# Expert tiles that do not exist count nothing on any engine; the last MLP block holds the last 512 tokens in token order and is stored by plain transfers

## The reference

```
# 1. linear attention with a decaying state, per head h
state = gamma[h] * state + k_t^T v_t ;  y_t = (q_t @ state) / 8
# 2. mixture of experts, 8 experts, 512 -> 1024 -> 512, one expert per token
e = argmax(x @ w_gate)
out = softmax(x @ w_gate)[e] * sigmoid(x @ w_output_gate)[e] * (relu(x @ w1[e]) @ w2[e])
# 3. gated MLP on every token, 512 -> 1536 -> 512
xn = x / sqrt(mean(x*x) + 1e-6) * rms_g
result = (silu(xn @ w_gate) * (xn @ w_val)) @ w_out
```

## Time and profile before

| | us |
|---|---|
| timed runs, median (lowest to highest) | 1160.51 (1159.92 to 1163.32) |
| the profiled execution | 1156.39 |
| its span | 1154.6 |
| TensorE matmul busy | 1117.5, 97% of the span |
| VectorE, ScalarE, GpSimd busy | 437.6, 383.0, 166.0 |

### The profile page before, as it was taken

One profiled execution on the slowest core, in us unless ns is written; L12 is line 12 of the kernel. 1 busy time (PEld: TensorE's weight loads), 2 busy tenths in 40 slices (PEclk: granted clock), 3 DMA queues, 4 the chain that ended last, 5 costly groups with the idle time before them and its releaser, 6 DMA issues.

```text
span 1154.6 us, 19327 instructions
## 1 busy us (share of the span) xinstructions
PE 1117.5 (97%) x6051; PEld 936.4 (81%) x6052; DVE 437.6 (38%) x826; ACT 383.0 (33%) x631; POOL 166.0 (14%) x216
## 2 busy tenths in 40 slices
PE   7999999999999999998999999999999999999995
PEld 6999988787878887876888788888888888888884
DVE  4777755432414416331434323222332332333221
ACT  2455433443434436432241313213131321313111
POOL 2444423333311101110000100100010010001001
PEclk9999999999999999998999999999999999999998
DMA  9989814534334633422200200100010010000000
GB/s 206 254 231 241 215 56 155 178 114 127 109 109 139 207 109 110 159 81 90 84 26 1 74 1 1 73 0 0 0 73 0 0 73 0 0 0 37 1 1 36
DMA packets 111838, 97.24 MB, mean 84 GB/s; under 512 B 80640, under 2 KB 86192, under 8 KB 111792
## 3 DMA queue, kind: packets, MB, share of 16 engines
q1 hardware_dynamic: 97744, 66.07, 20.7%
q0 software_dynamic: 7648, 22.60, 5.5%
q10 hardware_dynamic: 6400, 7.96, 2.1%
HBM read 76.40 MB, written 20.21 MB: 84 GB/s over the span
## 4 chain that ended last, share of the span: by engine, by line
PE 52%; ACT 0%; DVE 0%; issue 0%; POOLq 0%; POOL 0%; ACTq 0%
PE bank L660 17%; PE bank L662 17%; PE bank L661 17%; PE bank L631 0%; DVE hl L1279 0%; ACT hh L936 0%; POOLq L97 0%; POOL out_rows L1446 0%; ACT more_rows L943 0%; POOLq L1450 0%; ACTq L935 0%; POOLq L1445 0%
## 5 line engine op out<-in xcount | busy, mean ns | idle before, releaser
L1270 DVE TENSOR_TENSOR gated<-bank,sig 128x512 f32<-128x512 f32 x72 | 49.8, 692 | 323.0 <-ACT sig L929 323.0
L660 PE MATMUL bank<-xh,w1h 128*128 128x512 f32 x384 | 149.4, 389 | 0.0
L661 PE MATMUL bank<-xl,w1h 128*128 128x512 f32 x384 | 149.4, 389 | 0.0
L662 PE MATMUL bank<-xh,w1l 128*128 128x512 f32 x384 | 149.4, 389 | 0.0
L929 ACT ACTIVATE sig<-bank 128x512 f32<-128x512 f32 x72 | 43.1, 598 | 289.7 <-PE bank L662 289.7
L660 PE MATMUL bank<-w2h,hh 128*128 128x512 f32 x288 | 113.2, 393 | 4.7 <-DVE hl L1279 4.7
L662 PE MATMUL bank<-w2h,hl 128*128 128x512 f32 x288 | 112.2, 390 | 0.0
L661 PE MATMUL bank<-w2l,hh 128*128 128x512 f32 x288 | 112.1, 389 | 0.0
L1088 DVE TENSOR_TENSOR hidl<-bank,hidh 128x512 fp32r<-128x512 f32 x58 | 39.8, 687 | 151.1 <-ACT hidh L804 151.1
L1446 POOL DMA_INDIRECT out_rows<-x_out,cur_idx x12 | 11.8, 982 | 591.1 <-ACT x_out L943 589.3
L936 ACT ACTIVATE hh<-prod 128x512 fp32r<-128x512 f32 x72 | 45.5, 632 | 154.2 <-PE bank L662 133.6
(11 more groups left out here) (214 smaller groups left out, 1966.8 us busy)
## 6 DMA issues: line engine op xcount, KB each, us to landing
stage<-in_moe_w SPq DMA_DIRECT2D x64, 512.0 KB, 5.3
expert_rows<-tile_o ACTq DMA_DIRECT2D x29, 256.0 KB
q_raw<-in_q SPq DMA_DIRECT2D x24, 256.0 KB, 5.5
k_raw<-in_k SPq DMA_DIRECT2D x24, 256.0 KB, 6.2
v_raw<-in_v SPq DMA_DIRECT2D x24, 256.0 KB, 3.5
yr<-expert_rows SPq DMA_DIRECT2D x5, 1024.0 KB, 5.7
stage<-in_moe_w_out SPq DMA_DIRECT2D x6, 512.0 KB, 3.3
stage<-in_moe_w_gate SPq DMA_DIRECT2D x5, 512.0 KB, 7.1
```

Of the source, the lines that this page charges most:

```text
L660: pe.matmul(out_ap, lh, rh, start=first, stop=False)
L661: pe.matmul(out_ap, lh, rl, start=False, stop=False)
L662: return pe.matmul(out_ap, ll, rh, start=False, stop=last)
L1270: v3.tensor_tensor(gated[:], bank[GV[f % 2][0]][:, :], sig[:], ALU.mult).then_inc(s["gated_done"], 1)
```

## The change

- **Tiles that do not exist.** TensorE and ScalarE lose their Else branches and count nothing for a missing tile. A third word of `flags`, `extra`, holds the number of real tiles beyond 24. Each waiter loads it and waits for `extra + SURE` tiles. ScalarE's result of the last real tile moves behind the loop. TensorE's first down product waits for `tile_out` (the bank has been read) in place of `tile_stored`.
- **Order of the rows in the MLP.** Blocks 0 to 4 hold the tokens of units 0 to 19, packed by expert; block 5 holds units 20 to 23 in token order. A row's place in `expert_rows` is now a third word of its metadata, and every block is fetched by four indirect DMAs of GpSimd (`fetch_y`, `fetch_late`) in place of plain ones. For block 0 these wait for 17 stored tiles in place of 13, and stand ahead of `fetch_rows(20)` in place of `fetch_rows(19)`.
- **Metadata.** 20 units are scattered in place of 24, two behind each of the fetches of tiles 6 to 15, and read back behind the fetch of tile 17 in place of tile 18. Routing gains four small VectorE instructions ahead of `control_ready`, three ahead of `gates_ready`, and two copies behind it.
- **Stores.** Blocks 0 to 4 are stored as before. Block 5 is stored by four plain DMAs of SyncE, one for each `sum_out`.

The diff, cut to its core:

```diff
-ROWS_FROM = SURE - 5
-FINAL_AFTER = 13
+ROWS_FROM = SURE - 4
+FINAL_AFTER = 17
...
-        meta_dram = nc.dram_tensor("row_meta", (TOKENS, 2), U32).ap()
+        meta_dram = nc.dram_tensor("row_meta", (LEAD_UNITS * P, 3), U32).ap()
...
-            def load_rows(n):
-                sp.wait_ge(s["xn_turned"], KD * n)
-                sp.dma_start(yr[:].bitcast(U32), y_dram[ds(n * BLK * P, BLK * P), :].rearrange("(t p) d -> p t d", p=P))\
-                  .then_inc(s["yrows_in"], 16)
-
-            sp.wait_ge(s["tile_stored"], 16 * TILES)
-            with sp.Fori(1, NBLK) as n:
-                load_rows(n)
+            extra = sp.value_load(flags[0:1, 2:3], min_val=0, max_val=TILES - SURE)
+            sp.wait_ge(s["tile_stored"], 16 * (extra + SURE))
+            sp.sem_inc(s["stood"], 1)
             for t in range(BLK):
-                sp.wait_ge(out_stored[t], 16 * NBLK)
+                sp.wait_ge(s["sum_out"], BLK * (NBLK - 1) + t + 1)
+                sp.dma_start(out[(LEAD_UNITS + t) * P:(LEAD_UNITS + t + 1) * P, :], out_rows(t))\
+                  .then_inc(s["late_stored"], 16)
+            sp.wait_ge(s["late_stored"], 16 * BLK)
+            for t in range(BLK):
+                sp.wait_ge(out_stored[t], 16 * (NBLK - 1))
...
-                with pe.Else():
-                    pe.wait_ge(s["tiles_done"], a + 1)
-                    pe.sem_inc(s["tiles_done"], 1)
...
+            extra = pe.value_load(flags[0:1, 2:3], min_val=0, max_val=TILES - SURE)
...
-                    pe.wait_ge(s["tile_stored"], 16 * TILES)
+                    pe.wait_ge(s["tile_out"], extra + SURE)
+                    pe.sem_inc(s["stood"], 1)
...
-                    act.wait_ge(s["rows0_in"], 32)
+                    act.wait_ge(s["rows0_in"], 16 * BLK)
                 else:
-                    act.wait_ge(s["yrows_in"], 16 * n)
...
-            def result_if_real(a):
-                with act.If(act.value_load(real[0:1, ds(a, 1)], min_val=0, max_val=1)):
-                    tile_result(a)
-                    store_tile(a)
-                with act.Else():
-                    act.wait_ge(s["tile_stored"], 16 * a)
-                    act.sem_inc(s["tile_stored"], 16)
...
                     expert_tile(a)
-                with act.Else():
-                    result_if_real(a - 1)
 
             with act.Fori(SURE, TILES - 1) as a:
                 tile_if_real(a)
             tile_if_real(TILES - 1)
-            result_if_real(TILES - 1)
+            extra = act.value_load(flags[0:1, 2:3], min_val=0, max_val=TILES - SURE)
+            tile_result(extra + SURE - 1)
+            store_tile(extra + SURE - 1)
...
-            settle(v3.tensor_tensor_scan(upto_n[:], scan_ones[:], n_e[:], 0.0, ALU.mult, ALU.add))
-            settle(v3.tensor_tensor(ahead_e[:], upto_n[:], n_e[:], ALU.subtract))
+            also(v3.tensor_tensor(early_n[:], lead_counts, ecap, ALU.subtract))
+            settle(v3.tensor_tensor_scan(upto_n[:], scan_ones[:], n_e[:], 0.0, ALU.mult, ALU.add), 2)
+            also(v3.tensor_tensor_scan(early_upto[:], scan_ones[:], early_n[:], 0.0, ALU.mult, ALU.add))
+            settle(v3.tensor_tensor(ahead_e[:], upto_n[:], n_e[:], ALU.subtract), 2)
+            also(v3.tensor_tensor(early_e[:], early_upto[:], lead_counts, ALU.subtract))
...
-            settle(v3.tensor_scalar(flags[:, 0:1], runs_f, -2.0, None, ALU.add), 6)
+            also(v3.tensor_scalar(flags[:, 2:3], end_e[0:1, EXPERTS - 1:EXPERTS], float(LEAD - SURE), None, ALU.add))
+            settle(v3.tensor_scalar(flags[:, 0:1], runs_f, -2.0, None, ALU.add), 7)
...
+                also(v3.tensor_tensor(order[:], onehot[:, 0:LEAD_UNITS, :],
+                                      early_e[:, :].unsqueeze(1).to_broadcast([P, LEAD_UNITS, EXPERTS]), ALU.mult))
                 settle(v3.tensor_tensor(back[:], onehot[:], back_e[:, :].unsqueeze(1).to_broadcast([P, UNITS, EXPERTS]),
-                                        ALU.mult), 2)
-                settle(v3.tensor_reduce(back_f[:], back[:], X, ALU.add))
-                settle(v3.tensor_tensor(meta_idx[:], slot_f[:], back_f[:], ALU.add))
+                                        ALU.mult), 3)
+                also(v3.tensor_reduce(order_f[:], order[:], X, ALU.add))
+                settle(v3.tensor_reduce(back_f[:], back[:], X, ALU.add), 2)
+                also(v3.tensor_tensor(meta_idx[:], slot_f[:, 0:LEAD_UNITS], order_f[:], ALU.add))
+                settle(v3.tensor_tensor(meta[:, :, 2].bitcast(U32), slot_f[:], back_f[:], ALU.add), 2)
                 dve.sem_inc(s["gates_ready"], 1)
+                v3.tensor_copy(row_scale[:, LEAD_UNITS:], meta[:, LEAD_UNITS:, 0]).then_inc(s["late_set"], 1)
+                v3.tensor_copy(late_y[:], meta[:, LEAD_UNITS:, 2].bitcast(U32)).then_inc(s["late_set"], 1)
...
-            dve.wait_ge(s["tiles_done"], TILES + 1)
+            extra = dve.value_load(flags[0:1, 2:3], min_val=0, max_val=TILES - SURE)
+            dve.wait_ge(s["tiles_done"], extra + SURE + 1)
...
+            def fetch_y(n):
+
+                first = isinstance(n, int) and n == 0
+                for t in range(BLK):
+                    if not isinstance(n, int):
+                        pool.wait_ge(s["yrows_in"], 16 * BLK * (n - 1))
+                    nc.gpsimd.tensor_copy(cur_y4[:, t:t + 1], meta_back[:, ds(BLK * n + t, 1), 2].bitcast(U32))\
+                        .then_inc(s["y_staged"], 1)
+                if not first:
+                    pool.wait_ge(s["xn_turned"], KD * n)
+                pool.wait_ge(s["y_staged"], BLK * (n + 1))
+                pool.sem_inc(s["stood"], 1)
+                for t in range(BLK):
+                    nc.gpsimd.indirect_dma_start(block_rows(n, t).bitcast(U32), None, y_dram,
+                                                 bass.IndirectOffsetOnAxis(cur_y4[:, t:t + 1], 0))\
+                      .then_inc(s["rows0_in" if first else "yrows_in"], 16)
+
+            def fetch_late():
+
+                pool.wait_ge(s["late_set"], 2)
+                pool.wait_ge(s["xn_turned"], KD * (NBLK - 1))
+                for t in range(BLK):
+                    nc.gpsimd.indirect_dma_start(block_rows(NBLK - 1, t).bitcast(U32), None, y_dram,
+                                                 bass.IndirectOffsetOnAxis(late_y[:, t:t + 1], 0))\
+                      .then_inc(s["yrows_in"], 16)
...
-            for i in range(UNITS // 3):
+            for i in range(LEAD_UNITS // 2):
                 fetch_rows(LEAD + 4 + i)
-                for u in range(3 * i, 3 * i + 3):
+                for u in range(2 * i, 2 * i + 2):
                     scatter_meta(u)
-            assert LEAD + 4 + UNITS // 3 <= ROWS_FROM
-            with pool.Fori(LEAD + 4 + UNITS // 3, ROWS_FROM) as a:
+            assert LEAD + 4 + LEAD_UNITS // 2 <= ROWS_FROM - 2
+            with pool.Fori(LEAD + 4 + LEAD_UNITS // 2, ROWS_FROM - 2) as a:
                 fetch_rows(a)
 
-            pool.wait_ge(s["meta_stored"], 16 * UNITS)
-            with nc.allow_non_contiguous_dma(reason="two words to a row"):
+            pool.wait_ge(s["meta_stored"], 16 * LEAD_UNITS)
+            with nc.allow_non_contiguous_dma(reason="three words to a row"):
                 pool.dma_start(meta_back[:].bitcast(U32), meta_dram.rearrange("(j p) c -> p j c", p=P))\
                   .then_inc(s["meta_in"], 16)
+            with pool.Fori(ROWS_FROM - 2, ROWS_FROM) as a:
+                fetch_rows(a)
             pool.wait_ge(s["tile_stored"], 16 * FINAL_AFTER)
             pool.wait_ge(s["early_done"], 2)
-            pool.dma_start(x_rows[:].bitcast(U32), y_dram[0:2 * P, :].rearrange("(t p) d -> p t d", p=P))\
-              .then_inc(s["rows0_in"], 16)
-            pool.dma_start(more_rows[:].bitcast(U32), y_dram[2 * P:4 * P, :].rearrange("(t p) d -> p t d", p=P))\
-              .then_inc(s["rows0_in"], 16)
             pool.wait_ge(s["meta_in"], 16)
-            nc.gpsimd.tensor_copy(out_idx[:], meta_back[:, :, 1].bitcast(U32)).then_inc(s["ids_ready"], 1)
-
+            fetch_y(0)
             with pool.Fori(ROWS_FROM, SURE) as a:
                 fetch_rows(a)
             with pool.Fori(SURE, TILES) as a:
 
                 with pool.If(pool.value_load(real[0:1, ds(a - 1, 1)], min_val=0, max_val=1)):
                     fetch_rows(a)
...
+            extra = pool.value_load(flags[0:1, 2:3], min_val=0, max_val=TILES - SURE)
+            pool.wait_ge(s["tile_stored"], 16 * (extra + SURE))
+            pool.sem_inc(s["stood"], 1)
+            fetch_y(1)
             store_block(0)
-            with pool.Fori(1, NBLK) as n:
+            with pool.Fori(1, NBLK - 2) as n:
+                fetch_y(n + 1)
                 store_block(n)
+            fetch_late()
+            store_block(NBLK - 2)
```

(29 more changed lines are left out.)

4 lines of the change are left out of this document (2 added, 2 removed).

## The result

| | before | after |
|---|---|---|
| timed runs, median (lowest to highest), us | 1161.45 (1159.92 to 1163.32) | 1147.8 (1145.86 to 1149.8) |
| the profiled execution | 1156.39 | 1147.4 |
| its span | 1154.6 | 1145.6 |
| end of the last matmul to the end of the span | 11.19 | 3.09 |

The ratio is 0.9882, interval [0.9858, 0.9906], from four runs of each kernel: faster by 1.2%. The forecast was 1151.1 us, its range 1147.0 to 1156.5, so the time lies 3.3 us under the forecast, near the range's lower end.

The account below looks back on a forecast made before the run. TensorE's matmuls, busy 1117.5 of 1154.6 us, bound the kernel, so only its hole behind tile 28 and the end could pay: 2.3 + 7.1 = 9.4 us, 1160.5 to 1151.1 us, range 1147.0 to 1156.5.

Parts of the forecast that it names:

- The hole, 2.3 us: TensorE between tile 28 and the MLP: without the wait, the first matmul starts at 536.3, not 538.56; gain 2.3 us.
- What is late next: ScalarE at block 0: its table load comes early enough, the sigmoid 7.4 us behind the first matmul; no stall.
- The slow clock behind the hole, gain 0: Start of block 0: the lower clock still costs 1.7 us after a shorter hole, judged by tile 22; gain 0.
- The end, 7.1 us: Behind the last matmul: SyncE's plain stores land by 1147.0, span ends at 1147.5; gain 7.1 us, bounds 6.0 to 8.0.
- The drain: GpSimd's 9625 ns drain sets the program's end; about 100 us earlier it would be hidden, whatever it costs.
- the drain stays: Rival at the program's end: GpSimd's drain is long for another reason, only 2.3 us won, 1158.2 us; chance 0.11.
- Routing, GpSimd's queue, the gathers, at nothing: Added routing instructions, moved row fetches and fewer scatters all stay covered beside TensorE's work; cost 0.
- The cover of 2.4 us ahead of `fetch_rows(20)`: GpSimd's queue: block 0's gathers are issued by 393.3, while `fetch_rows(20)` was held by TensorE until 395.69; 2.4 us spare.
- a hole in tiles 18 to 20: Sign of being wrong: TensorE standing in these tiles, where the prediction expected no hole from tile 19 to 20.
- the rival of the collision: Block 0's gathers meet weight loads, ScalarE's stage piece comes late, TensorE stands: 4.0 us lost, 1155.1 us; chance 0.12.
- The offset: Timed median against profiled execution: the 4.1 us gap of the kernel before is taken for both kernels.

Follow-up runs that it names:

- skip_only: The kernel before with only the missing-tiles part of the change; row order, fetches and stores as before: 1157.45 us, ratio 0.9975.
- pe_counts: The changed kernel with TensorE's Else branch put back (wait for the tile before, add one), ScalarE still without: 1152.3 us, ratio 0.9932.
- before_drained: The kernel before with one GpSimd drain added between the stores of block 4 and those of block 5: 1152.01 us, ratio 0.9951.
- gp_copy: The changed kernel, with GpSimd waiting for the last result and then copying one column, no DMA: 1153.05 us, ratio 0.9941.
- after_again: The changed kernel itself, measured again against the kernel before in another session with more rounds: 1146.95 us, ratio 0.9911.
- gp_plain: The changed kernel with block 5's four plain stores issued by GpSimd instead of SyncE: 1154.33 us, ratio 0.9954.
- plain_drained: gp_plain with one GpSimd drain added ahead of its four plain stores of block 5: 1150.87 us, ratio 0.9931.
- gp_drain_first: gp_copy with a GpSimd drain added right behind the stores of block 4, ahead of the final copy: 1147.41 us, ratio 0.9914.

## Why the prediction was right

By its own steps:

- **The hole, 2.3 us.** Right, mechanism and size: 2.6 in the trace (5.75 to 3.17), 2.5 in skip_only's, 3.0 in its timed runs. An iteration was put at 1.4 us and takes 1.33; the load more was put at 0.75 and takes 0.65 (536.44 to 537.09). The matmul comes 3.2 us behind tile 28, against 536.3 - 532.81 = 3.5 forecast. The wait that falls away is 2.3 us by pe_counts.
- **What is late next.** ScalarE was not: its sigmoid waits only for TensorE, 7.4 us behind the first matmul, as forecast.
- **The slow clock behind the hole, gain 0.** Right: the clock fell again. The reason given, tile 22, is weaker than it looked. There TensorE stands 2.2 us in all eleven traces, and in 7 of 11 the clock fell behind it, in the changed kernel's not. That is worth about 1.4 us in a trace: from the end of that stop to the end of tile 28, before takes 532.81 - 446.28 = 86.5 us and before_drained, at the full clock, 532.85 - 447.75 = 85.1. (Tile 22 is seen in the window; the clock row of before's page shows only the place around 538 and the end of the span.)
- **The end, 7.1 us.** The mechanism was right, and its size is the mis-sized term: 8.1 us, just outside its bounds of 6.0 and 8.0. The span was to end at 1147.5 with the last `sum_out` at 1144.07, 3.4 us behind; it ended 2.5 us behind the last copy (1143.16 to 1145.6). The last landing was put 2.9 us behind the last copy, with room for four stores getting in each other's way; it came 2.1 us behind, as each took 2.0 us, also 0.7 us apart. The remaining waits and the barrier were put at 0.5 us and took 0.4.
- **The drain.** That it is hidden, "whatever a drain costs", held: 10.7 us in the shade. The reading behind it, a drain "5 us behind the last landing" that belonged to the stores just ahead, was half right. The price is due to transfers, but to those of the whole kernel: gp_copy paid it in full with the last one 96 us back, and before's 9.6 us are 2.8 of stores still queued and 6.8 of price. So the rival "the drain stays", which had "work of the whole queue that is only cleared at the end of the program", named the cause and still fell, because GpSimd reaches its drain early once it has nothing left to wait for. gp_copy is that rival made real: in its trace the end won 2.6 us, in the place of 8.1. The Trainium skill (VectorE: DVE Perf Modes, section The DRAIN you can't avoid) has these drains at "~12 ns constant". SyncE's 13 ns agrees; GpSimd's 280 to 10703 ns does not, nor do TensorE's 3.0 us, VectorE's 730 ns and ScalarE's 626 ns at the end, and the measurement decides.
- **Routing, GpSimd's queue, the gathers, at nothing.** Held but for a few tenths. The cover of 2.4 us ahead of `fetch_rows(20)` was 2.87, and the gathers went 1.26 us apart. But the prediction named a hole in tiles 18 to 20 as a sign of being wrong, and there is one of 0.47 us at tile 19, at the wait for a stage piece that the rival of the collision had named. It is 0.12 to 0.74 us, 0.45 on average, in the eight traces with the gathers, and 0, 0.13 and 0.13 us in the three without. So that rival came true at about a tenth of its price of 4.0 us.
- **The offset.** The step that failed: "the timed median is 4.1 us above that execution; I take the difference for both kernels". For the changed kernel it is 0.4. The profiled execution of before, 1156.39, lay at the low end of that kernel's 37 timed runs (1156.2 to 1163.32). The sum of the terms was 9.4 against 9.0 in the trace and 10.1 timed in the session of after_again; the 13.7 of the first comparison is that of four runs of each. That 9.4 lies so near 9.0 is luck in part. The two gains made 10.7 in the trace, and 2.0 us were lost again ahead of the hole, which the prediction had at nothing. As far as the table above can tell, those 2.0 are scatter.

## What to carry to other kernels

Read the row of each engine's last drain: where GpSimd has issued 100 transfers and more, its drain ends 6.5 to 7.8 us behind its last operation, and it belongs under other work, either by letting another engine make the last stores or by one explicit drain ahead of the last ones (one line, 5 us, in before_drained). Where a sequencer runs some 3.5 us ahead of its array and a question for each item that may be missing costs it 1.3 us, the third in a row stops the array (3.5 / 1.3, an estimate); give the loop its end as a number instead. Take the difference of two traces as the forecast of a difference, and don't carry the gap between one profiled execution and its timed runs from one kernel to the next.

## What was not expected of the hardware

- GpSimd's first drain behind its transfers ends 6.45 us behind the engine's last operation with 103 transfers ahead of it, 7.43 with 121, 7.76 with 125, and 7.45 with 121 of which the last was issued 96 us ago. With none since an earlier drain it took 280 ns, with four no longer than their landing.
- The length of a drain contains what its engine still has queued: TensorE's 3023 ns end 0.05 us behind its last matmul.
- Plain stores of 256 KB by SyncE took 0.33 to 0.36 us of issue and 2.0 us to landing, also 0.7 us apart. The same stores issued by GpSimd, in gp_plain, took 2.4 and 2.7 us to landing.
- The clock fell behind the same stop of 2.2 us at tile 22 in 7 of 11 traces, and behind a stop of 2.0 to 2.2 us at tile 4 in 3 of them (gp_copy, pe_counts, plain_drained). In skip_only and gp_drain_first, with 2.1 us at tile 4, it did not fall there. A window of gp_copy there:
```profile
218.00:221.00 3.00, 3.00 (x15) 2.71 (x14) 1.87 (x3) 1.86 (x4) 0.98 (x1) 0.55 0.00 0
```
  What decides it is open.
